# Where the networks' code stands: behind the attention's branch, or in each arm of it

## The chip, the cores and the metric

The kernel runs on one core of one Trainium2 chip. Time is the device time of one execution in microseconds. The kernel before was timed three times: 876.01, 876.82 and 877.76 us, median 876.82 us. Lower is better.

## The reference, cut to what matters

Three stages follow one another; the arrays are float32.

```python
def reference(q, k, v, n_sink, window, w_in, w_out, domain_probs, w1, w2):
    # 1 attention: batch 2, 8 heads, 768 positions, head size 64; scores q.k/8, kept where the
    #   key is one of the first n_sink or 0 <= i - j < window; softmax; times v
    x = attention.transpose(0, 2, 1, 3).reshape(1536, 512)
    # 2 first network: 512 -> 2048 -> 512
    h = x @ w_in
    x = (h * tanh(log1p(exp(min(h, 20))))) @ w_out
    # 3 second network: 4 experts, 512 -> 1024 -> 512, mixed by normalised domain_probs
    p = domain_probs / (domain_probs.sum(-1) + 1e-9)
    return sum(p[:, e:e+1] * (relu(x @ w1[e]) @ w2[e]) for e in range(4))
```

`n_sink` is 4 and `window` is 128 here, but both are inputs that the kernel reads while it runs.

## The kernel before, in words

Each engine has an instruction stream of its own, written out in the order in which it runs, and the engines meet through semaphores. Every weight and activation is split into two parts (`_hi` and `_lo`), so one product of matrices is three passes of TensorE (PE).

**The branch.** VectorE (DVE) works out a flag from `n_sink` and `window` (L1317). PE, ScalarE (ACT), DVE and GpSimd (POOL) each load it into a register and branch by it (L769, L1061, L1500, L473): where the flag is 1 they run `window_attention`, which computes only the blocks of scores near the diagonal and the sinks; otherwise `full_attention`, which computes all scores. With the inputs here every engine runs `window_attention`. The code of the other arm lies in the stream behind it and is jumped over; that jump is recorded under the line of the `If`, as its second execution. Behind the two arms, once in the stream of each engine, stands the code of both networks. The queue of SyncE (SP), which loads tiles and stores the output, has no such branch.

**The end of the attention.** `window_attention` ends with the start of the first network. On PE three `start_up` steps (L594, 12 passes each, 128x512) are laid between the last attention steps. On ACT it ends with `take_after` (L967, the copy of the last attention output to `x_hi`). On DVE it ends with its counterpart for `x_lo` (L1403). On POOL it ends with the scaling of probabilities (L443).

**The first network.** For each of 6 passes over 512 tokens (3 chunks, two groups of 8 tiles of the hidden layer) `chunk` alternates `up` (12 matmuls of L594 into one PSUM bank) and, three steps later, `down` (12 matmuls of L783). Between them stands the gate: DVE takes the bank (L1345), ACT an exponential (L945), DVE L1351, ACT a logarithm and an exponential (L949, L951), DVE four operations (L1361, L1364, L1371, L1377), ACT the high part (`gate_hi`, L1079), DVE the low part (`gate_lo`, L1514), and `down` waits for that (`mish_lo`). ACT also splits weight tiles (L958, L961), whose low part POOL completes by a DMA that adds (L439). The first thing that ACT does in the networks' code is such a split, L958; PE's first is the fourth `up`; DVE's is `gate_lo(0)`, which waits for ACT; POOL's is an add (L439), which waits for ACT. The last three passes on PE are a hardware loop (L803).

**The second network.** 16 pairs of hidden tiles by 2 halves of the tokens: `product` (L812, seven products in place of eight) and `tile_down` (L886), and DVE adds the results into the output accumulators (`evict`, L1655). Most of it is a hardware loop on every engine (L929 on PE, L1251 on ACT, L1716 on DVE). A loop's branch back is recorded under the loop's line.

**The end.** DVE's last `evict` frees the last output tile, SP stores it (L417) and waits for it to land. At L115 all five engines then meet: each drains and reports, POOL collects the reports and releases all.

Of the kernel before, what the change touches and what calls it, by code (L numbers as in the profile page):

```python
# [106 lines left out]
def build(nc, qT, kT, v, vs, params, weights, probs, out):  # L107
# [7 lines left out]
    with ExitStack() as ctx:  # L115
# [305 lines left out]
        def _(pl):  # L421
# [48 lines left out]

            pl.wait_ge(flag_ready, 1)
# [12 lines left out]

            def raw_blocks(p):
                r = 2 * (p % 2)
                return [w_raw[:, r + n, 2 * P * k:2 * P * (k + 1)] for n in range(2) for k in range(2)]

            def make_s1(p):

                for r in (2 * (p % 2), 2 * (p % 2) + 1):
                    pl.wait_ge(raw_in[r], 16 * ((FIRST + 2 * p) // RAW + 1))
                if p >= 2:
                    pl.wait_ge(w_sum_in, 16 * p)
                _, _, a21, a22 = raw_blocks(p)
                pl.tensor_tensor(sums_of(p)[:, 0, :], a21, a22, ALU.add).then_inc(w_sum_done, 1)

            def make_s2(p):
                pl.wait_ge(w_sum_done, 4 * p + 1)
                a11, _, _, _ = raw_blocks(p)  # L500
                pl.tensor_tensor(sums_of(p)[:, 1, :], sums_of(p)[:, 0, :], a11, ALU.subtract).then_inc(w_sum_done, 1)

            def make_s3(p):
                a11, _, a21, _ = raw_blocks(p)
                pl.tensor_tensor(a21, a11, a21, ALU.subtract).then_inc(w_sum_done, 1)

            def make_s4(p):
                pl.wait_ge(w_sum_done, 4 * p + 2)
                _, a12, _, _ = raw_blocks(p)
                pl.tensor_tensor(sums_of(p)[:, 2, :], a12, sums_of(p)[:, 1, :], ALU.subtract).then_inc(w_sum_done, 1)  # L510

            def add_tokens(s, name, count):

                pl.wait_ge(x_neg_done, count)
                source = rows(t_temp(s, name)) if name[0] == "T" else x2_block(s, int(name[1]) - 1, int(name[2]) - 1)
                pl.dma_start(rows(x_part(True, s, name)), source, accum_op=ALU.add).then_inc(x_added[s][name], 16)

            def add_sums(p):

                pl.wait_ge(w_neg_done, FIRST + 3 * p + (3 if p < 2 else 1))  # L520
                if p >= 1:
                    pl.wait_ge(w_sum_in, 16 * p)
                pl.dma_start(sum_cols(w_lo, p % 2), sums_of(p), accum_op=ALU.add).then_inc(w_sum_in, 16)  # L523

            def add_tile(p, n):

                r = 2 * (p % 2) + n
                pl.wait_ge(w_neg_done, FIRST + 3 * p + n + (1 if p < 2 else 2))
                pl.dma_start(w_cols(w_lo, p % 2 * SLOT + n * WC, WC), w_raw[:, r, :], accum_op=ALU.add)\
                    .then_inc(w_lo_in[r], 16)  # L530

            add_raw(EARLY - 1, (EARLY - 1) % RAW, EARLY)
            for t in range(NC * MISH):
                for f in range(STEPS):
                    for k, _ in splits(t, f):
                        add_raw(k % STEPS, k % RAW, (t // NC) * STEPS + k + 1)
            before_last, last = STEPS * (NC * MISH - 2), STEPS * (NC * MISH - 1)
            pl.wait_ge(g_done, before_last + 4)
            make_s1(0)
            pl.wait_ge(g_done, before_last + 5)  # L540
            make_s2(0)
            pl.wait_ge(g_done, before_last + 6)
            make_s3(0)
            pl.wait_ge(g_done, before_last + 7)
            make_s4(0)

            pl.wait_ge(g_done, last)
            make_s1(1)
            pl.wait_ge(g_done, last + 1)
            make_s2(1)  # L550
            pl.wait_ge(g_done, last + 2)
            make_s3(1)
            pl.wait_ge(g_done, last + 3)
            make_s4(1)
            add_tile(0, 0)
            add_tile(0, 1)
            add_tokens(0, "T1", 1)
            add_sums(0)
            add_tokens(0, "T2", 2)
            add_tokens(0, "T3", 3)  # L560
            add_tokens(0, "B22", 4)
            add_tile(1, 0)
            add_tile(1, 1)
            add_sums(1)
            add_tokens(1, "B21", 5)
            add_tokens(1, "B22", 6)

            pl.wait_ge(xc_lo, len(LO_ORDER[0]) + len(LO_ORDER[1]))
            for p in range(2, PAIRS):
                make_s1(p)  # L570
                make_s2(p)
                make_s3(p)
                make_s4(p)
                add_sums(p)
                add_tile(p, 0)
                add_tile(p, 1)

        @block.tensor
        def _(pe):
# [186 lines left out]

            pe.wait_ge(flag_ready, 1)
# [6 lines left out]
            def down(s, f, drained, by_bank=False):  # L774
                hidden_ready(s)
                g = f % G_RING
                for i in range(CT):
                    if f == 0 and drained is not None:

                        pe.wait_ge(bank_out, drained + i + 1)  # L780
                    lo, hi = CT * P + i * P, CT * P + (i + 1) * P
                    for n, (w, h) in enumerate(((w_hi, g_hi), (w_hi, g_lo), (w_lo, g_hi))):
                        mm = pe.matmul(banks[:, i, :], w[:, f, lo:hi], g_slot(h, g), start=(f == 0 and n == 0),  # L783
                                       stop=(f == STEPS - 1 and n == 2), skip_group_check=True)
                    if by_bank and i < CT - 1:
                        mm.then_inc(last_down, 1)
                mm.then_inc(down_done, 1)

            def chunk(t, c, before):
                for f in range(STEPS):  # L790
                    if before or f >= LAG:
                        up(t, c, t * STEPS + f, f, before)
                    if f >= LAG:
                        down(t * STEPS + f - LAG, f - LAG, (t - 1) * CT if before else None)
                    elif before:
                        down(t * STEPS + f - LAG, f - LAG + STEPS, None)


            pe.wait_ge(x_lo_done, X_DONE)
            chunk(0, 0, False)  # L800
            for t in range(1, NC):
                chunk(t, t, True)
            with pe.Fori(NC, NC * MISH) as t:  # L803
                chunk(t, t % NC, True)

            BANK_A, BANK_B, BANK_C = 4, 5, 7

            def product(bank, at, name, p2, s, first, last):

                for k in range(2):  # L810
                    for n, (w, lo) in enumerate(((w_hi, False), (w_hi, True), (w_lo, False))):
                        mm = pe.matmul(banks[:, bank, 0:HALF], w_cols(w, p2 * SLOT + at + k * P, P),  # L812
                                       x_part(lo, s, name)[:, k * HALF:(k + 1) * HALF],
                                       start=(first and k == 0 and n == 0), stop=(last and k == 1 and n == 2),
                                       skip_group_check=True)
                mm.then_inc(prod_done, 1)

            def tokens_ready(p, s, name):
                if isinstance(p, int) and p == 0 and name in ADDED[s]:
                    pe.wait_ge(x_added[s][name], 16)  # L820
                elif isinstance(p, int) and p == 0:
                    pe.wait_ge(xc_lo, len(LO_ORDER[0]) * s + LO_ORDER[s].index(name) + 1)

            def product_1(p, turn, p2, s):
# [116 lines left out]
        def _(act):  # L941
# [121 lines left out]
            with act.Else():  # L1063
                full_attention()
# [698 lines left out]
```

## Time and profile before

| what | value |
|---|---|
| median of 3 runs | 876.82 us |
| the profiled execution's own time | 877.44 us |
| its span, first to last instruction | 875.6 us |
| outside the span | 1.84 us |
| PE / DVE / ACT / POOL busy | 858.6 / 614.7 / 401.6 / 170.0 us |
| granted clock of TensorE | 1.00 in every slice |

The span is shown in slices of 21.9 us; PE is at 6 to 9 tenths in the first five (the attention), at 9 tenths in nearly all others. The profile's "issue" is time in which an engine stood still for nothing that the profile shows: no semaphore and no transfer.

### The profile page before, as it was taken

How to read it: one execution, taken by the hardware profiler on the slowest of the kernel's cores; microseconds unless marked ns; L12 is line 12 of the kernel's file. 1: busy time of each engine (PE TensorE's matmuls, PEld its weight loads, DVE VectorE, ACT ScalarE, POOL GpSimd, SP SyncE). 2: the span in 40 equal slices, each digit the busy share in tenths (PEclk: the TensorE clock that was granted, in tenths of full speed). 3: DMA queues.
4: the chain of work that ended last, by engine and by line, in shares of the span. 5: the costliest groups of instructions: out<-in, count | busy, mean ns of one | idle time of the engine just before them, and what ended most of it. 6: DMA issues, size and time to landing. Idle time of an engine off the chain costs nothing.

```text
span 875.6 us, 13835 instructions
## 1 busy us (share of the span) xinstructions
PE 858.6 (98%) x4448; PEld 733.5 (84%) x4448; DVE 614.7 (70%) x1219; ACT 401.6 (46%) x739; POOL 170.0 (19%) x255
## 2 busy tenths in 40 slices
PE   6999989999999999999999999999999999999998
PEld 4666767888888888889989999889998899998897
DVE  5888759989898999985665655656566565565655
ACT  4878755444874455873233133134224313313410
POOL 4666510000110011221220122022022112202100
PEclk9999999999999999999999999999999999999999
DMA  7454642000681000780541352254055135313303
GB/s 250 126 132 115 155 108 66 0 1 1 133 203 49 0 0 6 164 167 1 115 102 34 93 114 49 64 114 87 26 114 114 28 86 114 58 56 66 66 1 144
DMA packets 25192, 72.72 MB, mean 83 GB/s; under 512 B 4288, under 2 KB 5952, under 8 KB 25152
## 3 DMA queue, kind: packets, MB, share of 16 engines
q0 software_dynamic: 10720, 33.82, 21.2%
q1 hardware_dynamic: 14288, 38.04, 13.2%
q10 hardware_dynamic: 144, 0.39, 0.2%
q8 instruction: 17, 0.28, 0.1%
q14 instruction: 23, 0.19, 0.1%
HBM read 35.28 MB, written 3.15 MB: 44 GB/s over the span
## 4 chain that ended last, share of the span: by engine, by line
PE 92%; ACT 3%; DVE 2%; issue 1%; DMA 0%; DVEq 0%; POOL 0%; ACTq 0%
PE banks L886 30%; PE banks L812 27%; PE banks L783 14%; PE banks L594 14%; PE banks L609 2%; PE banks L680 2%; ACT pool L972 2%; PE banks L650 2%; PE banks L661 1%; DMA prm<-params 0%; ACT pool L949 0%; DVE g_lo L1514 0%; DVE pool L1423 0%; ACT w_hi L958 0%; ACT pool L951 0%
## 5 line engine op out<-in xcount | busy, mean ns | idle before, releaser
L1655 DVE SCALAR_TENSOR_TENSOR pool<-banks,p_norm,pool 128x512 f32<-128x512 f32 x180 | 133.6, 749 | 66.6 <-PE banks L886 64.8
L886 PE MATMUL banks<-w_hi,g_lo 128*128 128x512 f32 x384 | 150.6, 392 | 0.0
L886 PE MATMUL banks<-w_lo,g_hi 128*128 128x512 f32 x384 | 150.5, 392 | 0.0
L886 PE MATMUL banks<-w_hi,g_hi 128*128 128x512 f32 x384 | 149.3, 389 | 0.0
L1196 ACT ACTIVATE g_hi<-pool 128x384 fp32r<-128x384 f32 x96 | 50.5, 526 | 190.8 <-DVE pool L1635 139.2
L812 PE MATMUL banks<-x_hi,w_lo 128*128 128x384 f32 x256 | 85.9, 336 | 0.0
L812 PE MATMUL banks<-x_hi,w_hi 128*128 128x384 f32 x256 | 85.9, 335 | 0.0
L812 PE MATMUL banks<-x_lo,w_hi 128*128 128x384 f32 x256 | 85.7, 335 | 0.0
L886 PEld LDWEIGHTS banks<-w_hi,g_lo 128*128 128x128 f32 x384 | 72.1, 188 | 15.1
L886 PEld LDWEIGHTS banks<-w_lo,g_hi 128*128 128x128 f32 x384 | 72.1, 188 | 13.9
L886 PEld LDWEIGHTS banks<-w_hi,g_hi 128*128 128x128 f32 x384 | 72.1, 188 | 13.6
L783 PE MATMUL banks<-g_hi,w_hi 128*128 128x512 f32 x192 | 75.6, 394 | 1.8 <-DVE g_lo L1514 1.8
L594 PE MATMUL banks<-x_hi,w_hi 128*128 128x512 f32 (+1 forms) x192 | 75.1, 391 | 1.4 <-issue 1.4
L1190 ACT ACTIVATE g_hi<-banks 128x384 fp32r<-128x384 f32 x32 | 15.7, 491 | 131.3 <-PE banks L812 131.3
L523 POOL DMA_DIRECT2D w_lo<-w_sum x15 | 13.1, 875 | 323.2 <-ACT w_lo L1106 323.2
L783 PE MATMUL banks<-g_hi,w_lo 128*128 128x512 f32 x192 | 74.8, 390 | 0.0
L783 PE MATMUL banks<-g_lo,w_hi 128*128 128x512 f32 x192 | 74.8, 390 | 0.0
L594 PE MATMUL banks<-x_hi,w_lo 128*128 128x512 f32 (+1 forms) x192 | 74.7, 389 | 0.0
L594 PE MATMUL banks<-x_lo,w_hi 128*128 128x512 f32 (+1 forms) x192 | 74.7, 389 | 0.0
L1642 DVE SCALAR_TENSOR_TENSOR g_lo<-pool,g_hi 128x384 fp32r<-128x384 f32 x96 | 53.3, 556 | 21.6 <-ACT g_hi L1196 17.8
L949 ACT ACTIVATE pool<-pool,two 128x512 f32<-128x512 f32 x48 | 34.8, 725 | 70.0 <-DVE pool L1351 69.9
L443 POOL TENSOR_TENSOR pool<-pool,row_den 128x272 f32<-128x272 f32 (+2 forms) x96 | 54.6, 594 | 39.2 <-DVE row_den L1396 39.0
(134 smaller groups left out, 1752.0 us busy)
## 6 DMA issues: line engine op xcount, KB each, us to landing
w_raw<-weights SPq DMA_DIRECT2D x48, 512.0 KB, 4.3
w_lo<-w_raw POOLq DMA_DIRECT2D x48, 512.0 KB, 5.4
w_lo<-w_sum POOLq DMA_DIRECT2D x15, 384.0 KB, 4.0
pool<-kT SPq DMA_DIRECT2D x8, 400.0 KB, 4.4
pool<-v SPq DMA_DIRECT2D x8, 384.0 KB, 3.2
out<-pool SPq DMA_DIRECT2D x12, 256.0 KB, 2.0
pool<-qT SPq DMA_DIRECT2D x7, 384.0 KB, 3.2
w_lo<-pool POOLq DMA_DIRECT2D x2, 384.0 KB, 4.9
```

What stands on the lines that cost most here:

```text
L443: pl.tensor_tensor(p, p, inverse.to_broadcast([P, width]), ALU.mult).then_inc(prob_ready, 1)
L594: mm = pe.matmul(banks[:, 4 + f % H_RING, :], w[:, f, k * P:(k + 1) * P], x[:, k, ds(c * CHUNK, CHUNK)], start=(k == 0 and n == 0), stop=( ...
L609: mm = pe.matmul(bank[:, col:col + n], q_pair[rows, b, j * P:(j + 1) * P], k_pair[rows, b, key:key + n], start=True, stop=True)
L650: mm = pe.transpose(banks[:, TURN_BANK + n, P * (2 * h + k):P * (2 * h + k) + P], window_prob(u + h, WIDE)[:, col:col + P], ident[:, :])
L680: mm = pe.matmul(banks[D * h:D * h + D, out_bank, column], v_pair[:, b, kt, D * h:D * h + D], prob_T[:, slot, P * (2 * h + k):P * (2 * h + ...
L783: mm = pe.matmul(banks[:, i, :], w[:, f, lo:hi], g_slot(h, g), start=(f == 0 and n == 0), stop=(f == STEPS - 1 and n == 2), skip_group_che ...
L812: mm = pe.matmul(banks[:, bank, 0:HALF], w_cols(w, p2 * SLOT + at + k * P, P), x_part(lo, s, name)[:, k * HALF:(k + 1) * HALF], start=(fir ...
L886: mm = pe.matmul(banks[:, bank, :], g[:, s, f * SUP + at:f * SUP + at + P], w_cols(w, p2 * SLOT + DOWN_AT[f], DM), start=(f == 0 and n == ...
L949: act.activation(r_buf[:, s % 2, :], n_buf[:, s % 2, :], ACT.Ln, bias=two[:, 0:1]).then_inc(l_done, 1)
L1196: act.activation(relu_of(s, f, l), source, ACT.Relu).then_inc(relu_hi, 1)
L1642: dve.scalar_tensor_tensor(out=g_lo[:, s, at], in0=source, scalar=0.0, in1=g_hi[:, s, at].bitcast(f32), op0=ALU.max, op1=ALU.subtract).the ...
L1655: dve.scalar_tensor_tensor(out=to, in0=d_bank, scalar=share, in1=to, op0=ALU.mult, op1=ALU.add)\
```

## The change

On each of the four engines that branch, everything that stood behind the two arms (both networks, with their loops) becomes a function `networks()`, and that is called at the end of each arm. The body of `networks()` is what stood there, line by line, with a deeper indent. SP's stream is not changed, nor are the waits, the tiles and the order on any engine. Each stream now has the code of the networks twice; the one that lies in the other arm isn't run. GpSimd's part in full but for the body, and the other three by their branches:

```diff
@@ gpsimd
+            def networks():
+                def raw_blocks(p):
...
+                add_raw(EARLY - 1, (EARLY - 1) % RAW, EARLY)
...
             pl.wait_ge(flag_ready, 1)
             small = pl.value_load(flag[0:1, 0:1])
             with pl.If(small == 1):
                 window_attention()
+                networks()
             with pl.Else():
                 pl.iota(prob[:, 0, :], ...
                 full_attention()
-            def raw_blocks(p):
...
-            add_raw(EARLY - 1, (EARLY - 1) % RAW, EARLY)
...
+                networks()
@@ tensor
             with pe.If(small == 1):
                 window_attention()
+                networks()
             with pe.Else():
                 full_attention()
+                networks()
@@ scalar
             with act.If(small == 1):
                 window_attention()
+                networks()
             with act.Else():
                 full_attention()
+                networks()
@@ vector
             with dve.If(small == 1):
                 window_attention()
+                networks()
             with dve.Else():
...
                 full_attention()
                 steps[0] = before
+                networks()
```

So the jump over the other arm, which stood between the attention and the networks, now stands between the last instruction of the networks and the meeting at L115.

## Rows read from the trace of the kernel before

**Rows 1.** The page's head and part 1: busy time, share, instructions.
```profile
span 875.6 us, 13835 instructions
PE 858.6 (98%) x4448; PEld 733.5 (84%) x4448; DVE 614.7 (70%) x1219; ACT 401.6 (46%) x739; POOL 170.0 (19%) x255
```

**Rows 2.** Waits, 112 to 136 us: engine, line, releaser, us, times, longest.
```profile
ACT w_hi L958 <- issue: 4.0, 1, 4.0
...
PE banks L783 <- DVE g_lo L1514: 1.6, 3, 0.8
PE banks L594 <- issue: 1.4, 1, 1.4
```

**Rows 3.** Branches by source line: ns min/median/max, first and last start.
```profile
L769 PEldq COMPARE_BRANCH  x2: 80/2421/4762, 7.3 to 111.7; - x2
...
L1061 ACTq COMPARE_BRANCH  x2: 40/44/47, 7.1 to 112.4; - x2
...
L1500 DVEq COMPARE_BRANCH  x2: 47/48/50, 8.5 to 112.8; - x2
...
L473 POOLq COMPARE_BRANCH  x2: 38/42/45, 7.1 to 104.3; - x2
```

**Rows 4.** Timeline of ACT: start us, us, engine, line, operation, idle before.
```profile
112.37 0.39 ACT L967 ACTIVATE x_hi<-banks 128x256 fp32r<-128x256 f32 x1 [3.34 <-PE banks L680]
116.70 1.06 ACT L958 ACTIVATE w_hi<-w_raw 128x1024 fp32r<-128x1024 f32 x1 [3.95 <-issue]
```

**Rows 5.** DMA queues, 112 to 116 us: packets, MB, share of 16 engines.
```profile
q8 instruction: 2, 0.03, 4.5%
q14 instruction: 2, 0.02, 1.6%
```

**Rows 6.** Timeline of POOL.
```profile
105.03 0.88 POOL L439 DMA_DIRECT2D w_lo<-w_raw  x1 [0.47 <-ACT w_lo L961]
```

**Rows 7.** Timeline of DVE.
```profile
119.27 0.69 DVE L1514 TENSOR_TENSOR g_lo<-pool,g_hi 128x512 fp32r<-128x512 f32 x1 [6.06 <-ACT g_hi L1079]
```

**Rows 8.** Timeline of PE around the end of the attention.
```profile
112.25 0.50 PE L594 MATMUL banks<-x_hi,w_hi 128*128 128x512 f32 x1
...
116.71 0.47 PE L594 MATMUL banks<-x_hi,w_hi 128*128 128x512 f32 x1 [1.42 <-issue]
...
132.82 0.50 PE L783 MATMUL banks<-g_hi,w_hi 128*128 128x512 f32 x1 [0.75 <-DVE g_lo L1514]
```

**Rows 9.** The chain of waits: start us, us, what.
```profile
132.07 0.70 DVE g_lo L1514
...
138.57 2.72 PE banks L783 x12
```

**Rows 10.** Stretches: length, busy by engine (count), clock, DMA share, GB/s.
```profile
136.00:160.00 24.00, 24.00 (x108) 19.87 (x107) 23.14 (x43) 12.57 (x21) 0.00 (x0) 1.00 0.05 18
...
480.00:840.00 360.00, 360.00 (x1804) 325.50 (x1803) 213.43 (x349) 117.05 (x183) 61.91 (x79) 1.00 0.35 77
```

**Rows 11.** Source line L115, the meeting at the end, columns as in rows 3.
```profile
L115 PEldq DRAIN  x1: 4267/4267/4267, 868.1 to 868.1; - x1
L115 DVEq DRAIN  x1: 789/789/789, 872.4 to 872.4; - x1
...
L115 SPq DRAIN  x1: 13/13/13, 875.4 to 875.4; - x1
```

**Rows 12.** Loop branches by source line, columns as in rows 3.
```profile
L803 PEldq COMPARE_BRANCH  x3: 76/216/247, 273.6 to 360.8; - x3
...
L929 PEldq COMPARE_BRANCH  x7: 76/208/211, 471.0 to 844.7; - x7
...
L1716 DVEq COMPARE_BRANCH  x7: 50/56/80, 476.1 to 849.9; - x7
```

**Rows 13.** DMA queues, 475 to 730 us: all that moved.
```profile
q0 software_dynamic: 3562, 11.86, 25.7%
q1 hardware_dynamic: 2304, 8.39, 9.8%
```

More of the change, by code:

```diff
@@ L469, in full_attention, with make_s1, make_s2, make_s3 @@
                     add_raw(k, k, k + 1)
+            def networks():
+                def raw_blocks(p):
+                    r = 2 * (p % 2)
+                    return [w_raw[:, r + n, 2 * P * k:2 * P * (k + 1)] for n in range(2) for k in range(2)]
+                def make_s1(p):
+                    for r in (2 * (p % 2), 2 * (p % 2) + 1):
+                        pl.wait_ge(raw_in[r], 16 * ((FIRST + 2 * p) // RAW + 1))
+                    if p >= 2:
+                        pl.wait_ge(w_sum_in, 16 * p)
+                    _, _, a21, a22 = raw_blocks(p)
+                    pl.tensor_tensor(sums_of(p)[:, 0, :], a21, a22, ALU.add).then_inc(w_sum_done, 1)
+                def make_s2(p):
+                    pl.wait_ge(w_sum_done, 4 * p + 1)
+                    a11, _, _, _ = raw_blocks(p)
+                    pl.tensor_tensor(sums_of(p)[:, 1, :], sums_of(p)[:, 0, :], a11, ALU.subtract).then_inc(w_sum_done, 1)
+                def make_s3(p):
+                    a11, _, a21, _ = raw_blocks(p)
+                    pl.tensor_tensor(a21, a11, a21, ALU.subtract).then_inc(w_sum_done, 1)
+                def make_s4(p):
+                    pl.wait_ge(w_sum_done, 4 * p + 2)
+                    _, a12, _, _ = raw_blocks(p)
+                    pl.tensor_tensor(sums_of(p)[:, 2, :], a12, sums_of(p)[:, 1, :], ALU.subtract).then_inc(w_sum_done, 1)
+                def add_tokens(s, name, count):
+                    pl.wait_ge(x_neg_done, count)
+                    source = rows(t_temp(s, name)) if name[0] == "T" else x2_block(s, int(name[1]) - 1, int(name[2]) - 1)
+                    pl.dma_start(rows(x_part(True, s, name)), source, accum_op=ALU.add).then_inc(x_added[s][name], 16)
+                def add_sums(p):
+                    pl.wait_ge(w_neg_done, FIRST + 3 * p + (3 if p < 2 else 1))
+                    if p >= 1:
+                        pl.wait_ge(w_sum_in, 16 * p)
+                    pl.dma_start(sum_cols(w_lo, p % 2), sums_of(p), accum_op=ALU.add).then_inc(w_sum_in, 16)
+                def add_tile(p, n):
+                    r = 2 * (p % 2) + n
+                    pl.wait_ge(w_neg_done, FIRST + 3 * p + n + (1 if p < 2 else 2))
+                    pl.dma_start(w_cols(w_lo, p % 2 * SLOT + n * WC, WC), w_raw[:, r, :], accum_op=ALU.add)\
+                        .then_inc(w_lo_in[r], 16)
+                add_raw(EARLY - 1, (EARLY - 1) % RAW, EARLY)
+                for t in range(NC * MISH):
+                    for f in range(STEPS):
+                        for k, _ in splits(t, f):
+                            add_raw(k % STEPS, k % RAW, (t // NC) * STEPS + k + 1)
+                before_last, last = STEPS * (NC * MISH - 2), STEPS * (NC * MISH - 1)
+                pl.wait_ge(g_done, before_last + 4)
+                make_s1(0)
+                pl.wait_ge(g_done, before_last + 5)
+                make_s2(0)
+                pl.wait_ge(g_done, before_last + 6)
+                make_s3(0)
+                pl.wait_ge(g_done, before_last + 7)
+                make_s4(0)
+                pl.wait_ge(g_done, last)
+                make_s1(1)
+                pl.wait_ge(g_done, last + 1)
+                make_s2(1)
+                pl.wait_ge(g_done, last + 2)
+                make_s3(1)
+                pl.wait_ge(g_done, last + 3)
+                make_s4(1)
+                add_tile(0, 0)
+                add_tile(0, 1)
+                add_tokens(0, "T1", 1)
+                add_sums(0)
+                add_tokens(0, "T2", 2)
+                add_tokens(0, "T3", 3)
+                add_tokens(0, "B22", 4)
+                add_tile(1, 0)
+                add_tile(1, 1)
+                add_sums(1)
+                add_tokens(1, "B21", 5)
+                add_tokens(1, "B22", 6)
+                pl.wait_ge(xc_lo, len(LO_ORDER[0]) + len(LO_ORDER[1]))
+                for p in range(2, PAIRS):
+                    make_s1(p)
+                    make_s2(p)
+                    make_s3(p)
+                    make_s4(p)
+                    add_sums(p)
+                    add_tile(p, 0)
+                    add_tile(p, 1)
@@ L483, in _ @@
                 full_attention()
-            def raw_blocks(p):
[L486 to L496, printed above, removed]
@@ L512, in add_tokens @@
[L512 to L523, printed above, removed]
@@ L525, in add_tile @@
[L525 to L530, printed above, removed]
-            add_raw(EARLY - 1, (EARLY - 1) % RAW, EARLY)
[L533 to L550, printed above, removed]
@@ L568, in _ @@
[L568 to L576, printed above, removed]
+                networks()
         @block.tensor
@@ L770, in _ @@
                 window_attention()
+                networks()
             with pe.Else():
                 full_attention()
[L774 to L824, printed above, removed]
-                it = 2 * p + s
-                if not isinstance(it, int) or it >= 1:
-                    pe.wait_ge(relu_lo, 4 * it - 3)
-                pe.wait_ge(w_lo_in[2 * p2], 16 * turn + 16)
-                tokens_ready(p, s, "B11")
-                product(BANK_A, A11, "B11", p2, s, True, False)
@@ L935, in _ @@
-            final = PAIRS - 1
-            pair_step(final, (FIRST + 2 * final) // RAW, 1, 1, final, 1)
-            for k in range(SUP_TILES):
-                tile_down(final, 1, 1, k)
+                networks()
         @block.scalar
@@ L1081, in x_hi_of @@
-            def x_hi_of(s, name):
-                if name[0] == "T":
-                    act.wait_ge(t_made, 4 * s + T_ORDER[s].index(name) + 1)
-                    act.wait_ge(up_done, STEPS * (NC * MISH - 1 + s))
-                    source = rows(t_temp(s, name))
-                else:
-                    if s == 0:
-                        act.wait_ge(bank_out, CT * (NC + 2 if name == "B22" else NC + 1))
-                    else:
-                        act.wait_ge(bank_out, CT * (NC * MISH - 1) + 2 * int(name[1]))
-                        act.wait_ge(down_done, NC * MISH * STEPS)
-                    source = x2_block(s, int(name[1]) - 1, int(name[2]) - 1)
-                act.activation(rows(x_part(False, s, name)), source, ACT.Copy).then_inc(xc_hi, 1)
@@ L1096, in x_neg_of @@
-            def x_neg_of(s, name):
-                source = rows(t_temp(s, name)) if name[0] == "T" else x2_block(s, int(name[1]) - 1, int(name[2]) - 1)
-                act.activation(rows(x_part(True, s, name)), source, ACT.Copy, scale=-1.0).then_inc(x_neg_done, 1)
-            def sums_hi(p, p2):
-                act.wait_ge(w_sum_done, 4 * p + 4)
-                act.activation(sum_cols(w_hi, p2), sums_of(p), ACT.Copy)
-            def sums_neg(p, p2):
-                act.activation(sum_cols(w_lo, p2), sums_of(p), ACT.Copy, scale=-1.0).then_inc(w_neg_done, 1)
@@ L1192, in relu_sum @@
-            def relu_sum(it, s, n):
-                f, l, source = ((1, 1, c22), (0, 1, c12), (1, 0, c21))[n - 1]
-                act.wait_ge(sum_done, 5 * it + 2 + n)
-                act.activation(relu_of(s, f, l), source, ACT.Relu).then_inc(relu_hi, 1)
-            def relus(it, s):
-                relu_first(it, s)
-                for n in range(1, 4):
-                    relu_sum(it, s, n)
-            def next_weights(p, turn, p2):
-                act.wait_ge(tile_done, 2 * SUP_TILES * p - 2 * SUP_TILES)
-                sums_hi(p, p2)
-                sums_neg(p, p2)
-                tile_hi(p, turn, p2, 0)
-                tile_neg(p2, 0)
@@ L1266, in _ @@
-            for s in range(2):
-                copy_p1(2 * PAIRS - 2 + s)
-                relus(2 * PAIRS - 2 + s, s)
+                networks()
         @block.vector
@@ L1545, in x_lo_of @@
-            def x_lo_of(s, name):
-                dve.wait_ge(xc_hi, BLOCKS * s + HI_ORDER[s].index(name) + 1)
-                if s == 1 and name[0] == "T":
-                    dve.wait_ge(w_sum_in, 32)
-                source = rows(t_temp(s, name)) if name[0] == "T" else x2_block(s, int(name[1]) - 1, int(name[2]) - 1)
-                dve.tensor_tensor(rows(x_part(True, s, name)), source, rows(x_part(False, s, name)).bitcast(f32),
-                                  ALU.subtract).then_inc(xc_lo, 1)
@@ L1598, in _ @@
-            gate_lo(NC * MISH * STEPS - 2)
-            finish_first(NC * MISH * STEPS - 1)
-            finish_second(NC * MISH * STEPS - 1)
-            def bank(n):
-                return banks[:, n, 0:HALF]
-            def halves_used(it, n):
-                if not isinstance(it, int) or it >= 1:
-                    dve.wait_ge(relu_lo, 4 * it - 4 + n)
-            def sum_16(it, s):
-                halves_used(it, 3)
-                dve.wait_ge(prod_done, 7 * it + (3 if isinstance(it, int) and it == 0 else 2))
-                dve.wait_ge(p1_copied, it + 1)
-                dve.tensor_tensor(c12, bank(5 + s), p1_sum, ALU.add).then_inc(sum_done, 1)
@@ L1645, in evict @@
-            def evict(it, s, e, first, k):
-                dve.wait_ge(tile_done, SUP_TILES * it + k + 1)
-                tile = TILE_ORDER[k]
-                to, d_bank = out_acc(s, tile), banks[:, (2 * s + k) % 4, :]
-                token = s * SUP_TILES + tile
-                share = p_norm[:, ds(e, 1), token:token + 1].rearrange("p a n -> p (a n)")
-                if first:
-                    dve.tensor_scalar(to, d_bank, share, None, ALU.mult).then_inc(evicted, 1)
-                else:
-                    dve.scalar_tensor_tensor(out=to, in0=d_bank, scalar=share, in1=to, op0=ALU.mult, op1=ALU.add)\
-                       .then_inc(evicted, 1)
@@ L1721, in _ @@
-            pair_step(2 * PAIRS - 1, 1, E - 1, False)
-            for k in range(SUP_TILES):
-                evict(2 * PAIRS - 1, 1, E - 1, False, k)
+                networks()
 def kernel(q, k, v, n_sink, window, moe_w_in, moe_w_out, moe2_domain_probs, moe2_w1, moe2_w2):
```

920 lines of the change are left out of this document (510 added, 410 removed).

## The prediction

> **What bounds the kernel now.** Read in this order: the busy shares, the waits around the end of the attention, the branch records, the timelines of ACT and PE there, and last the meeting at the end. PE is busy for 858.6 of 875.6 us, and from 136 us on it never stands still (24.00 us busy of 24.00, later 360.00 of 360.00) [rows 1, 10]. [...] So any microsecond that the change takes from a standstill of PE before 136 us moves all later work forward as a whole, and one put on PE behind that is paid in full.
>
> Between 112 and 136 us PE has two kinds of standstill: 1.4 us of "issue" ahead of the fourth `up`, and three waits for `gate_lo`, 1.6 us together. ACT has one "issue" idle of 4.0 us in the same place [rows 2]. The branch records explain both. ACT reaches its jump over the other arm at 112.4 us, and the record lasts only 47 ns, but the next ACT instruction starts at 116.70 us, with nothing to wait for: 3.95 us of idle behind a copy that began at 112.37 us [rows 3, 4]. PE reaches its jump at 111.7 us and that record itself lasts 4.76 us, to 116.46 us; PE had a queue of matmuls to work off and shows only the last 1.42 us of it [rows 3, 8]. In these four microseconds the instruction queues move four packets [rows 5]. So the jump makes an engine fetch its next code, and costs it about 4.3 us (ACT, 112.4 to 116.70) to 4.8 us (PE).
>
> [...]
>
> **The part taken away.** Behind `window_attention` the next instruction now follows in sequence, so ACT starts L958 at about 112.75 in place of 116.70 us, 3.95 us earlier. Does PE gain as much? DVE's `gate_lo(0)` waited 6.06 us for ACT and nothing else [rows 7], so the whole chain of gates moves with ACT. The last wait of PE ends at 132.82 us; what released it was DVE L1514 at 132.07 us, itself released by ACT's high part [rows 8, 9], and that chain would end 3.95 us earlier: 128.87 us. PE's own work allows that: from 112.25 to 132.82 us it has six groups of twelve matmuls, a group that waits for nothing takes 2.72 us [rows 9], so 16.3 us plus 0.1 for the start of the first: 128.7 us, 4.1 us earlier [rows 8]. The later of the two counts: **gain 3.95 us**. PE's first `up` itself comes 1.4 us earlier, its first `down` no longer waits, and the third `down` is the one late by 0.2 us.
> Bounds: at least the 3.0 us of standstill that the waits show (1.4 + 1.6) [rows 2], at most the 4.1 us of PE's own work. I take 3.95, as the gates limit. Nothing else is late: POOL's add and SP's loads wait for ACT and follow it. DVE's own jump, at 112.8 us, lies under the wait for ACT (its next record is at 119.27) and is worth nothing by itself [rows 3, 7]. POOL's jump, at 104.3 us, was cheap: its next operation starts at 105.03, 0.7 us later, of which 0.47 us is a wait [rows 3, 6].
>
> **The part added.** Each of the four engines now jumps over the other arm, which has become longer by the networks, ahead of its drain at L115. The cost is what the latest of them adds to the meeting. PE is at its drain at 868.1 us, with 4.27 us of matmuls still queued, to 872.4 us; SP is last, at 875.4 us [rows 11]. With a jump of 4.8 us PE is there by 872.9 us: hidden. ACT and POOL have less to do for the last pair than PE and are ahead of it: hidden. DVE is not hidden: its drain is issued at 872.4 us, when its last `evict` starts, 3.0 us ahead of SP's [rows 11]. With a jump of J in between, the meeting is J - 3.0 us later. DVE's jump in this trace is only bounded: below by POOL's 0.7 us, above by 119.27 - 112.8 = 6.5 us [rows 3, 6, 7]. The nearest rows are ACT's 4.3 and PE's 4.8 us; I take 4.5, so **cost 1.5 us**, with ends 0 (J under 3.0, SP's last store covers it) and 3.5 us.
>
> **Loops and the rest.** The networks' code moves in each stream, and the loops stand elsewhere against the pieces in which code is fetched. Here the branch back costs PE about 0.21 us, under a full queue, and DVE 0.06 us [rows 12], and between 475 and 730 us no instruction packet moves at all [rows 13]: all loop bodies stay held. I price the shift at nothing, as the cover for it (held code) doesn't depend on where in a piece a loop begins, so far as its body is held with room to spare; if it isn't, that is rival C. Waits, tiles and transfers are unchanged; the second copy of the code isn't run and costs only its place.
>
> **Sum.** 877.44 (the profiled execution; span 875.6 and 1.84 around it) - 3.95 + 1.5 = 874.99 us. That execution lies 0.62 us above the median of the three runs, 876.82, so the median to expect is 874.4 us, 2.45 us or 0.28% lower. The least that a measurement of this kernel can tell from no change is about 0.2%, 1.75 us. The forecast's own range: gain 4.1, cost 0: 872.7; gain 3.0, cost 3.5: 877.3.
>
> **The rivals.**
> - A, the end is free: DVE's jump hides under the last store. That wants J under 3.0 us. For: POOL's jump cost 0.7 us at most. Against: POOL jumped over a short arm, DVE jumps over a whole copy of attention and networks. 876.82 - 3.95 = 872.9 us.
> - B, the gain is only PE's own: ACT's idle is not the jump's, or the gates turn late by something else, and only the 1.42 us of PE's "issue" goes, while the end still pays 1.5. For: one trace, one jump per engine, and "issue" is a name for what isn't seen. Against: ACT's and PE's idle have one time and one length, and PE's is in the branch record itself [rows 3, 4]. 876.9 us. With it stands the case that the jump never cost anything and nothing changes: 876.8 us.
> - C, slower: a loop that was held is held no more after the shift, and PE fetches at each branch back. There are 8 taken ones (2 of the 3 records of L803, 6 of the 7 of L929) [rows 12]. Each would be a fetch as at the jump, of which PE's queue left 1.42 us showing [rows 8]: 8 x 1.42 = 11.4 us, 874.4 + 11.4 = 885.8 us. It decides from 0.5 us per turn on, where it eats 2.45 + 1.75 us. For: the code does shift. Against: rows 12 and 13, loops of very different lengths held on PE and DVE.
> - D, the end costs twice: behind the meeting the engines run on, outside the span, in code that was prefetched in sequence and that after a jump must be fetched once more; another 4.3 us in place of nothing: 878.7 us. For: 1.84 us outside the span that no row explains. Against: after ACT's jump at 112.4 us no second gap follows [rows 2].
>
> [...]
>
> **How the numbers follow.** Forecast 0.62, A 0.10, B with no change 0.13, C 0.06, D 0.09. Faster by over 0.2% means under 875.07: four fifths of the forecast (J up to about 5.1) and all of A, 0.60. B and the rest of the forecast are within 0.2%, 0.25. C and D are slower, 0.15. The range that leaves out C, the upper half of D and the very edge of A is 872.6 to 878.2 us.
>
> **What would show it.** In the changed kernel's profile: no "issue" idle ahead of ACT L958 and PE L594 near 112 us; ACT's L958 starts within 0.1 us of the end of L967; the last wait of PE for `gate_lo` ends at about 128.9 us; all later PE groups are 3.95 us earlier, and DVE's last `evict` starts at 868.4 us. A branch record of DVE then stands there, its drain comes at about 872.9 us and SP's at 871.4, so DVE, not SP, is last at L115; the span is about 873.1 us. Wrong it would be if PE's branch-back records grew above 0.3 us, if instruction packets appeared in the loops, or if DVE's drain came within 3.0 us of the last `evict` (A) or more than 5.1 us behind it.

## The result, and the profile after

| | before | after |
|---|---|---|
| median of 7 runs each (lowest to highest) | 876.82 us (876.01 to 877.76) | 874.23 us (873.23 to 874.49) |
| ratio | | 0.9971, interval 0.9961 to 0.9981 |
| the profiled execution, its span | 877.44, 875.6 us | 874.49, 872.7 us |
| outside the span | 1.8 us | 1.8 us |

The change makes the kernel 2.6 us (0.29%) faster; 874.4 us was forecast. In the profile it is 4.1 us gained behind the attention and 1.2 us given back at the end. The second of these has another cause than the one forecast.

The lines of the kernel have shifted with the edit: the branches are L939 (PE), L1272 (ACT), L1724 (DVE), L567 (POOL); `up` is L597, `down` L780, the splits L964 and L967, the copy of x L973, `gate_lo` L1511, `evict` L1652.

First, page head and busy times of after [rows 1]:

```profile
span 872.7 us, 13835 instructions
PE 857.5 (98%) x4448; PEld 733.7 (84%) x4448; DVE 614.7 (70%) x1219; ACT 401.4 (46%) x739; POOL 170.0 (19%) x255
```

Where the 4.1 us come from: the waits of after between 112 and 136 us [rows 2] have no `issue` idle of ACT any more and none of PE before a matmul, only one of 0.2 us before a weight load.

```profile
ACT x_hi L973 <- PE banks L683: 3.3, 1, 3.3
DVE g_lo L1511 <- ACT g_hi L1079: 2.0, 1, 2.0
PEld banks L780 <- DVE g_lo L1511: 0.3, 1, 0.3
PEld banks L597 <- issue: 0.2, 1, 0.2
```

The timelines of ACT, DVE and PE of after in the same place (start us, length us, engine, line, operation, idle before it) [rows 4, 7, 8]:

```profile
112.37 0.39 ACT L973 ACTIVATE x_hi<-banks 128x256 fp32r<-128x256 f32 x1 [3.34 <-PE banks L683]
112.65 1.05 ACT L964 ACTIVATE w_hi<-w_raw 128x1024 fp32r<-128x1024 f32 x1
...
115.20 0.69 DVE L1511 TENSOR_TENSOR g_lo<-pool,g_hi 128x512 fp32r<-128x512 f32 x1 [1.99 <-ACT g_hi L1079]
...
112.25 0.50 PE L597 MATMUL banks<-x_hi,w_hi 128*128 128x512 f32 x1
115.13 0.39 PE L597 MATMUL banks<-x_hi,w_hi 128*128 128x512 f32 x1
...
128.76 0.50 PE L780 MATMUL banks<-g_hi,w_hi 128*128 128x512 f32 x1
```

The copy of the last x begins at 112.37 us in both profiles, so these rows compare directly. ACT's first split starts 4.05 us sooner (116.70 to 112.65), the fourth `up` 1.58 us sooner, and the third `down`, the last that waited before, 4.06 us sooner (132.82 to 128.76) and with no wait. From there the gain is carried to the end: DVE's last `evict` waits for PE as before and starts 4.09 us sooner (872.40 to 868.31).

```profile
868.31 0.75 DVE L1652 SCALAR_TENSOR_TENSOR pool<-banks,p_norm,pool 128x512 f32<-128x512 f32 x1 [0.61 <-PE banks L883]
```

The jump itself is where it was put: each branch's second record is now at the end [rows 3]. The view is that of the branch records by source line (ns shortest/middle/longest, first and last start in us); with them the drains of L115 [rows 11].

```profile
L939 PEldq COMPARE_BRANCH  x2: 89/1984/3880, 7.4 to 864.1; - x2
L1272 ACTq COMPARE_BRANCH  x2: 38/42/45, 7.2 to 860.8; - x2
L1724 DVEq COMPARE_BRANCH  x2: 47/48/50, 8.5 to 868.3; - x2
...
L115 ACTq DRAIN  x1: 80/80/80, 863.4 to 863.4; - x1
L115 PEldq DRAIN  x1: 328/328/328, 868.0 to 868.0; - x1
L115 DVEq DRAIN  x1: 71/71/71, 871.5 to 871.5; - x1
L115 SPq DRAIN  x1: 13/13/13, 872.5 to 872.5; - x1
```

A jump's price is read as the drain's start less the branch's: ACT 2.6 us, DVE 3.2 us, PE 3.9 us. DVE reaches its drain at 871.5 us, ahead of SP: it is not last. SP is, as before, but 1.2 us later than its work should allow: from the last `evict` to the end of the span it is 3.2 us before (872.40 to 875.6) and 4.4 us after (868.31 to 872.7). What grew is the landing of the last store. Its issue in the stretch 869 to 873 us of after (queues: packets, MB, share of 16 engines; then the issue, KB, us to landing), and behind the dots the stretch 870.9 to 872.0 us alone:

```profile
q1 hardware_dynamic: 211, 0.37, 24.8%
q8 instruction: 1, 0.02, 1.5%
q14 instruction: 2, 0.02, 1.0%
...
out<-pool SPq DMA_DIRECT2D x1, 256.0 KB, 3.2
...
DMA  0100100100200100100100100100101000000000
...
q1 hardware_dynamic: 14, 0.02, 5.4%
```

The same stretch around the last store of the kernel before, 873 to 876 us:

```profile
q1 hardware_dynamic: 226, 0.40, 35.4%
...
out<-pool SPq DMA_DIRECT2D x1, 256.0 KB, 2.0
```

The store takes 3.2 us in place of 2.0, and in its last microsecond packets of the store alone move, one after the other, at the tenths that one of 16 DMA engines gives: fifteen are done and one is late. That it is one DMA engine is read from the share (5.4% of 16 engines) and the even spacing; the trace doesn't name the engine. The new company of the store is the code that PE fetches when it resumes behind its jump (868.0 us): one packet of 16 KB on q8, which by its record starts at 869.22 us and takes 0.98 us, as long as twelve of the store's packets of 2 KB (0.08 us each). Two packets of 8 KB on q14, DVE's by their time, move there too (869.6 and 872.1 us); e3 and e5 tell the two apart.

The loops are as before [rows 10, 12, 13]: branch back and stretches of after (length, busy by engine, clock, DMA share, GB/s).

```profile
L926 PEldq COMPARE_BRANCH  x7: 76/215/228, 466.9 to 840.7; - x7
L1713 DVEq COMPARE_BRANCH  x7: 50/56/69, 472.0 to 845.8; - x7
...
480.00:830.00 350.00, 350.00 (x1755) 316.54 (x1754) 207.12 (x339) 114.40 (x179) 59.12 (x76) 1.00 0.35 77
```

### The profile page after: what moved, and what is told of

Read it like the earlier page. It is cut to its first block, busy times and chain, and to the rows that moved or that the text cites. A ratio compares the mean times of both kernels' runs of the same rounds, so it can differ in the third digit from the quotient of the medians.

```text
span 872.7 us, 13835 instructions
## 1 busy us (share of the span) xinstructions
PE 857.5 (98%) x4448; PEld 733.7 (84%) x4448; DVE 614.7 (70%) x1219; ACT 401.4 (46%) x739; POOL 170.0 (19%) x255
## 3 DMA queue, kind: packets, MB, share of 16 engines
HBM read 35.28 MB, written 3.15 MB: 44 GB/s over the span
## 4 chain that ended last, share of the span: by engine, by line
PE 96%; ACT 1%; DVE 1%; issue 1%; DMA 1%; POOL 0%; DVEq 0%; ACTq 0%
PE banks L883 30%; PE banks L809 27%; PE banks L780 15%; PE banks L597 15%; PE banks L612 3%; PE banks L683 2%; PE banks L653 2%; ACT pool L978 1%; PE banks L664 1%; DMA prm<-params 1%; DVE pool L1432 0%; DVE mask L1303 0%; DVE pool L1392 0%; PE banks L651 0%; POOL pool L443 0%
## 5 line engine op out<-in xcount | busy, mean ns | idle before, releaser
L1652 DVE SCALAR_TENSOR_TENSOR pool<-banks,p_norm,pool 128x512 f32<-128x512 f32 x180 | 133.6, 749 | 66.7 <-PE banks L883 64.9
L780 PE MATMUL banks<-g_hi,w_hi 128*128 128x512 f32 x192 | 75.3, 392 | 0.2 <-DVE g_lo L1511 0.2
L597 PE MATMUL banks<-x_hi,w_hi 128*128 128x512 f32 (+1 forms) x192 | 75.0, 391 | 0.0
L780 PE MATMUL banks<-g_hi,w_lo 128*128 128x512 f32 x192 | 74.8, 390 | 0.0
L780 PE MATMUL banks<-g_lo,w_hi 128*128 128x512 f32 x192 | 74.8, 389 | 0.0
L597 PE MATMUL banks<-x_hi,w_lo 128*128 128x512 f32 (+1 forms) x192 | 74.7, 389 | 0.0
L597 PE MATMUL banks<-x_lo,w_hi 128*128 128x512 f32 (+1 forms) x192 | 74.7, 389 | 0.0
```

The source lines that it names most:

```text
L597: mm = pe.matmul(banks[:, 4 + f % H_RING, :], w[:, f, k * P:(k + 1) * P], x[:, k, ds(c * CHUNK, CHUNK)], start=(k == 0 and n == 0), stop=( ...
L1652: dve.scalar_tensor_tensor(out=to, in0=d_bank, scalar=share, in1=to, op0=ALU.mult, op1=ALU.add)\
```

## The experiments

Each kernel's time stands against the kernel before in the same series (its medians there: 876.41 for e1, e2, e3 and e5, 876.62 for e4 and e6 to e8, 876.67 for e9 to e11). The end of the attention falls up to a microsecond earlier or later from run to run (the copy of the last x at 111.4 to 113.4 us in these profiles), so the profiles are split at two points that don't depend on it. **Way**: from the start of that copy to the start of the last `evict`. **Tail**: from there to the end of the span. The last store is given from its issue to its landing. Each kernel has one profile, so way, tail and store are one execution's.

| kernel | way, us | tail, us | last store, us | median | less before | ratio, interval |
|---|---|---|---|---|---|---|
| before | 760.03 | 3.2 | 2.0 | 876.82 | | |
| after | 755.94 | 4.4 | 3.2 | 874.23 | -2.59 | 0.9971, 0.9961 to 0.9981 |
| e11, after again | 755.98 | 4.3 | 3.2 | 874.17 | -2.50 | 0.9975, 0.9966 to 0.9985 |
| e1, ACT only | 757.67 | 3.2 | 2.0 | 874.30 | -2.11 | 0.9975, 0.9963 to 0.9986 |
| e2, PE only | 758.47 | 3.7 | 2.5 | 876.76 | +0.35 | 1.0001, 0.9992 to 1.0010 |
| e3, DVE and POOL | 759.60 | 3.4 | 2.2 | 876.59 | +0.18 | 1.0000, 0.9991 to 1.0009 |
| e4, all but PE | 757.77 | 3.3 | 2.1 | 874.94 | -1.68 | 0.9981, 0.9972 to 0.9990 |
| e5, PE and ACT | 756.46 | 4.5 | 3.3 | 874.74 | -1.67 | 0.9980, 0.9971 to 0.9989 |
| e6, hint late | 758.63 | 3.2 | 2.0 | 875.70 | -0.92 | 0.9989, 0.9980 to 0.9998 |
| e7, hint late, DVE too | 758.47 | 3.2 | 2.0 | 875.62 | -1.00 | 0.9988, 0.9979 to 0.9997 |
| e8, after, PE's end hinted | 755.99 | 3.4 | 2.3 | 873.47 | -3.15 | 0.9962, 0.9948 to 0.9975 |
| e9, and DVE's end | 755.95 | 3.4 | 2.2 | 874.10 | -2.57 | 0.9974, 0.9963 to 0.9985 |
| e10, before, hint early | 756.23 | 3.2 | 2.0 | 873.39 | -3.28 | 0.9963, 0.9950 to 0.9977 |

The profiled execution of before was 0.62 us above its median. If that excess lies in its way and tail, they overstate a gain against the medians by as much; with it taken off, the two agree within 0.4 us in all but e2 and e9 (by 0.8 and 0.7 us). The intervals of the ratios are some 1 us wide to each side, so differences of 1 us or less between two of the kernels are read from the profiles and not from the medians.

Theory 1, after the two traces: the way is ACT's and PE's jump, and the tail is PE's code fetch in the way of the last store. Theory 2: the tail is DVE's jump, as forecast, or DVE's fetch.

**e1, e2 and e3: one engine's part alone.** The networks stay behind the branch on the engines that are not named; on them, as here on PE for e1:

```diff
             with pe.If(small == 1):
                 window_attention()
-                networks()
             with pe.Else():
                 full_attention()
-                networks()
+            networks()
```

> The networks stand inside the arms on ACT alone; PE, DVE and POOL as before. Theory 1 (the gates set the gain, and at the end PE's code fetch delays the last store): PE keeps its jump and resumes at 116.7 us, then runs five groups without a wait, so its third down starts at 116.71 + 2.83 + 4 x 2.72 = 130.4 in place of 132.82 us, 2.4 us earlier, and the end costs nothing: 876.8 - 2.4 = 874.4 us, last store landed in 2.0 us. Theory 2 (DVE's jump is what costs at the end) gives the same here. Rival 3 (each engine's idle counts by itself, PE's 1.4 and ACT's remainder 2.6): 874.2 us.

> The networks stand inside the arms on PE alone. Theory 1: PE's fourth up starts 1.6 us earlier, but the gates wait for ACT's jump as before, the third down stays at 132.8 us, nothing is gained; at the end PE's code fetch meets the last store, which lands in 3.2 in place of 2.0 us: 876.8 + 1.2 = 878.0 us. Theory 2 (DVE's jump costs at the end): 876.8 us. Rival 3 (PE's own idle counts by itself): 1.4 us less at the start, 875.4 us, with or without 1.2 at the end.

> The networks stand inside the arms on DVE and POOL alone. Theory 1: nothing at the start (both jumps lie under waits), and at the end DVE's drain comes 3.15 us after its last evict, about when SP's does: 876.8 to 877.0 us, last store landed in 2.0 us. Theory 2: DVE's code fetch delays the last store: 878.0 us with a landing of 3.2 us.

e1 came at -2.1 us, with the tail of before: ACT's part alone carries most of the gain and nothing of the cost. What it leaves is PE's own idle, 1.5 us here.

```profile
PE banks L597 <- issue: 1.5, 1, 1.5
```

e2 was expected 1.2 us above before and came level, a miss. Its way is 1.6 us shorter though ACT still jumps: where PE doesn't jump, ACT's jump is shorter too. The timeline of ACT in e2 and the third `down` of PE:

```profile
115.11 1.06 ACT L964 ACTIVATE w_hi<-w_raw 128x1024 fp32r<-128x1024 f32 x1 [2.34 <-issue]
...
131.22 0.50 PE L780 MATMUL banks<-g_hi,w_hi 128*128 128x512 f32 x1 [0.75 <-DVE g_lo L1511]
```

ACT starts 2.7 us after the jump in place of 4.3. At the end PE's code packet (871.14 us, 1.06 us long) ends 1.3 us after the last `evict` begins, against 1.7 to 2.0 us in after, e11 and e5: here it meets the store before the last, which takes 3.2 us, and the last one takes 2.5. So what PE's jump costs at the end depends on where its fetch falls. That the median shows none of the 1.6 us beside a tail that is only 0.5 us longer is not explained by this profile.

e3 is the test of theory 2. DVE's jump is at the end, PE's is not; DVE's drain comes 0.1 us ahead of SP's, and the tail grows by 0.2 us, not by 1.2:

```profile
L115 DVEq DRAIN  x1: 70/70/70, 875.1 to 875.1; - x1
L115 SPq DRAIN  x1: 13/13/13, 875.2 to 875.2; - x1
```

DVE's jump of 3.1 us just fits under the last store, and the 0.2 us are the store's own (2.2 us in place of 2.0), with DVE's packet of 8 KB 0.6 us ahead of its first packet. Theory 2 falls as the account of the 1.2 us. DVE's own jump at the start was worth little beside the others: the way is 0.4 us shorter, with ACT's idle 3.60 in place of 3.95 us, and the median shows nothing.

**e5 and e4: what the parts do together.** The same edit, with PE and ACT inside, and with all but PE inside.

> The networks stand inside the arms on PE and ACT, not on DVE and POOL. Theory 1: the whole gain of 4.06 us at the start, and PE's code fetch still delays the last store by 1.2 us: 876.8 - 4.06 + 1.2 = 873.9 us, as with all four engines. Theory 2: the gain without the cost, 872.8 us, last store landed in 2.0 us. Both: the third down of PE at 128.8 us.

> The networks stand inside the arms on ACT, DVE and POOL, not on PE. PE resumes behind its own jump at 116.5 us or up to 1.6 us sooner, if the fetches of ACT and DVE are what lengthens it; then five groups without a wait. With PE's jump unchanged at 4.8 us: third down at 130.4, 2.4 us gained, and at the end only DVE's jump of 3.1 us, which ends with SP's drain: 876.4 - 2.4 + 0.1 = 874.1 us. If the end's cost were DVE's: 875.3 us.

In e5 the tail is the longest of all (4.5 us, last store 3.3 us, PE's fetch at 868.99 us taking 1.76 us), with DVE's jump not at the end at all: PE's part brings it without DVE's. The median, 874.7 us, is 0.8 us above the 873.9 expected. At the start DVE's jump now shows: it takes 2.8 us (112.7 to 115.55 us), `gate_lo(0)` is 0.35 us later than in after, and the third `down` waits for it again, 0.29 us:

```profile
129.11 0.50 PE L780 MATMUL banks<-g_hi,w_hi 128*128 128x512 f32 x1 [0.29 <-DVE g_lo L1511]
```

So the jump that was worth next to nothing with ACT's in place is worth 0.4 us without it: it is the next delay behind ACT's. In e4 PE jumps alone and takes 5.0 us, 1.7 of it past its queue; the other engines' jumps are not what makes PE's long. The tail is 3.3 us without PE's jump in it. The median, 874.9 us, is 0.8 us above the 874.1 expected.

**e8 and e11: the code fetched ahead.** The hint of these kernels gives a branch an earlier place in the stream (`mark_branch_hint_location`, `branch_hint`); that the fetch of its target can begin there was the author's assumption, and what it does is read from the runs (PE's jump at the end takes 3.9 us in after and 0.46 us in e8). e8 is the changed kernel with such a hint for PE's jump at the end, ahead of its last six `tile_down`; e11 is the changed kernel as it is.

```diff
+                hint_at[0] = pe.mark_branch_hint_location()
                 for k in range(SUP_TILES):
...
             with pe.If(small == 1):
+                behind = nc.cur_bb.bb.name.replace("_true", "_end")
                 window_attention()
                 networks()
+                pe.br(behind).branch_hint(hint_at[0])
```

> The changed kernel with a prefetch hint on PE's jump at the end, placed ahead of its last six output tiles. Theory 1 (PE's second fetch, at 869.2 us, delays the last store by sharing one DMA engine with it): PE jumps without a stall near 864 us, its fetches lie before 867 us, the last store lands in 2.0 us, and the end costs nothing: 0.5 to 1.2 us below the changed kernel, 872.4 us where before is 876.4. Theory 2 (DVE's fetch at 869.6 us delays it): landing stays at 3.2 us, no gain, 873.8 us.

> The changed kernel once more, in one job with its two relatives. All theories: 0.3% below before (0.2 to 0.4%), last store landed in 2.5 to 3.3 us, third down of PE 16.5 us after the first start_up pass of the third start_up.

PE's jump at the end falls from 3.9 to 0.46 us. Its two code packets start at 861.3 and 866.3 us, so none moves during the jump (865.1 us), and none is under the last store, whose packets are done after 2.3 us. The branch of PE in e8:

```profile
L945 PEldq COMPARE_BRANCH  x1: 457/457/457, 865.1 to 865.1; - x1
```

The tail is 3.4 us, against 4.3 and 4.4 us in the two profiles of the changed kernel: the cost of the tail is gone, with PE's jump and its fetch moved and nothing else changed. A store of 3.1 us is still there (the longest of the twelve), near the packet at 866.3 us, but it isn't the last. The median is 0.65 us further below the kernel before than e11's; the two intervals overlap, and it missed the 872.4 us expected by 1.1.

**e9: DVE's jump hinted too.** The same edit again on DVE, ahead of its loop over the second network.

> The changed kernel with hints on the end jumps of PE and of DVE. Theory 1: with PE's late fetch gone the last store lands in 2.0 us and SP would reach the meeting 3.0 us behind DVE's last evict; DVE's jump of 3.1 us is then as late as SP, so its hint is worth at most 0.2 us beside PE's hint alone. The whole 4.06 us of the start stay: 0.95 to 1.2 us below the changed kernel in this job, about 0.4% below the kernel before. If the end's cost had another source, equal to the changed kernel.

DVE's jump shrinks to 0.64 us, its drain comes 2.5 us ahead of SP's, and the tail stays at 3.4 us, as it must where SP is last. The median came out with e11's and not with e8's, a miss (0.95 to 1.2 us below the changed kernel was expected), though the profiled execution itself was at 873.37 us. So the tail is shown by the profiles; that the medians gain by it is not shown.

**e6 and e7: the hint on the kernel before, ten microseconds ahead.** No code is copied; the jump behind the attention gets the hint, on PE ahead of `start_up(0)` and on ACT ahead of its last splits in the attention; in e7 on DVE ahead of `start_gate(0)` too.

> The kernel before, its code not copied; PE and ACT get a prefetch hint for their jump over the other arm, some ten microseconds ahead of it. If the whole price of the jump is the fetch of its target, ACT's idle of 3.95 and PE's of 1.42 us go, with only DVE's own jump left (gate_lo late by 0.3 to 0.4 us, as where PE and ACT alone had the networks inside), and nothing is added at the end: 876.4 - 3.7 = 872.7 us. If the jump costs by itself, whatever has been fetched, no change: 876.4 us.

> As e6_hint, with the hint on DVE's jump too. Fetch theory: the whole 4.06 us of the start and no cost at the end, 876.4 - 4.06 = 872.3 us, last store landed in 2.0 us, which is below both kernels. If the jump costs by itself: 876.4 us.

Both missed, by 3.0 and 3.3 us. No packet of PE's code moved ahead of the jump. Yet the hint did something: PE's jump takes 3.0 us in place of 4.8, ACT's 2.9 and 2.7 us in place of 4.3, the way is 1.4 to 1.6 us shorter, and the median 0.9 to 1.0 us lower. What went is one packet of PE's code: 16 of 16 KB in the whole execution in place of 17, and one in place of two right behind the jump (before: 112.33 and 112.77 us; e6: 112.03 us). A packet of 16 KB moves at this place in the kernels without a jump of PE there as well (112.48 us in after, 112.42 in e2), and such packets move where PE runs on without a gap (before: 152.50 and 181.92 us, with PE busy for 104.00 of 104.00 us from 136 us on). So the first of before's two is likely a fetch in sequence, of code that is then jumped over, and the jump's own comes behind it. That reading was not tested by itself.

**e10: the same hint, far earlier.** On PE and DVE it is the first thing in the arm, on ACT it stands about 45 us ahead of the jump.

```diff
             with pe.If(small == 1):
+                behind = nc.cur_bb.bb.name.replace("_true", "_end")
+                hint_at = [pe.mark_branch_hint_location()]
                 window_attention()
+                pe.br(behind).branch_hint(hint_at[0])
...
+                        if ct == CT - 2 and g == 3:
+                            hint_at[0] = act.mark_branch_hint_location()
```

> The kernel before, no code copied, with the hints on the jump behind the attention placed far ahead: on PE and DVE as the first instruction of the arm, on ACT some 70 instructions earlier than in e6_hint. There the hints brought no fetch ahead of the jump; if that was because no new piece of code was fetched between hint and jump, the targets are now fetched early, the jumps cost under 0.5 us and the start's whole 4.06 us are gained without any cost at the end: 0.46% below before. If a fetched target is dropped again before the jump, or a hint ahead of a loop has no effect: as e6_hint, 0.1% below before.

ACT goes on 0.5 us after its jump, 0.2 us later than with no jump at all; PE's still takes 3.2 us, not under 0.5 as expected, but that lies under its queue. ACT's timeline and PE's branch in e10:

```profile
112.22 0.38 ACT L976 ACTIVATE x_hi<-banks 128x256 fp32r<-128x256 f32 x1 [3.35 <-PE banks L683]
112.72 1.06 ACT L967 ACTIVATE w_hi<-w_raw 128x1024 fp32r<-128x1024 f32 x1
...
L943 PEldq COMPARE_BRANCH  x1: 3211/3211/3211, 111.5 to 111.5; - x1
```

The way is 3.8 us shorter and the tail that of before: 873.39 us, the lowest median of all, 0.8 us under the changed kernel's in the same series (the intervals overlap), with the networks' code once in each stream. Against e8 (873.47 us, in another series) it is no different by these runs.

## Why the prediction was right

- **What bounds the kernel, and the gain of 3.95 us:** right; 4.06 us at the third `down` and 4.09 at the last `evict`. Of the two counts that were set against each other, PE's own work (4.1 us) was the one that held in the end: `gate_lo` was in time, and the third `down` has no wait. That ACT's jump is the larger part and PE's 1.4 us the smaller is e1's result.
- **The jump's price of 4.3 to 4.8 us:** right for the gaps it was read from, wrong as the price of a jump. ACT's is 2.7 us in e2 and 2.6 at the end of after, DVE's 2.8 in e5 and 2.9 to 3.2 at the end (e4, e3, after), PE's 3.8 (e2) and 3.9 at the end. Where two packets of PE's code move close together, ACT's is 4.0 to 4.3 us (e3, before), DVE's 4.0 (e1) and PE's own 4.8 to 5.0, alone too (e4).
- **DVE's J of 4.5 us, so 1.5 us at the end:** the term that was mis-sized. J is 3.2 us, so DVE's drain is 1.0 us ahead of SP's in place of 1.5 behind it, and 0.1 us ahead where PE doesn't jump (e3); DVE's part costs at most 0.2 us by itself, and that through the store (2.2 us in e3). POOL's 0.7 us, the lower bound that was given, was no price of a jump over the arm: its next operation starts at 105.05 us in after, with no jump, as against 105.03 before, and at the end its jump takes 3.8 us (820.6 to its drain at 824.4).
- **PE's jump at the end is hidden:** the step that failed. PE's drain is indeed early (868.0 us), but the cover was reckoned for the engine and not for the DMA that its jump starts. The fetch (0.98 us at 869.22 us) lies, by the reading of its packets above, in front of the last store's on one DMA engine, and the store is 1.2 us late. Shown by the store of 2.0 us in e1 and no more than 2.2 us in e3 and e4 (no PE jump at the end), 3.2 and 3.3 us in e11 and e5 (with it), and 2.3 us in e8 (with it, fetched early). In e2 the jump is there and the store takes 2.5 us, as the fetch falls earlier.
- **So the sum was right partly by luck:** 1.5 us for a reason that costs 0.2 stood in for 1.2 us of a reason priced at nothing. Without the second the sum gives rival A's 872.9 us. The profiles of e8 and e9 bear that out (way and tail together 3.8 us shorter than before's); their medians do so only in part (3.15 and 2.57 us lower, so 873.7 and 874.2 us against 876.82).
- **DVE's own jump at the start is worth nothing by itself:** right as said, within the 0.4 us by which e3's way is shorter; 0.4 us once ACT's is gone (e5), and the change has both.
- **POOL at nothing, loops at nothing (C), nothing behind the meeting (D):** right; branches back 215 and 56 ns, no instruction packet between 480 and 730 us, 1.8 us outside the span in both. That code is fetched ahead in sequence, as D has it, is seen on PE inside the span (packets at 152.50 and 181.92 us of before, under a PE without a gap); behind the meeting no trace shows it. B falls with e1.

## What to carry to other kernels

A branch over a long arm cost its engine 2.5 us (ACT at the end of e5) to 3.9 us (PE at the end of after) here, and up to 5.0 us (PE in e4) where two packets of PE's code moved at once, so look at what each engine is late for behind its jump, and price each with the others in place and with them gone. A jump that is hidden for its engine still moves code (16 KB at 869.2 us in after): look which transfer near it is the last one of the kernel. A hint far ahead of the branch gave at least the same gain here without a second copy of the code (e10: 873.39 us, e11: 874.17 us). Whether one worked is read from the gap behind the branch, engine by engine: packets of code ahead of it move with and without a hint (861.3 us in e8, 860.2 us in after).

## What the runs showed of the hardware that was not expected

- PE's jump is longer where two fetches of its code lie close together: it takes 4.8 to 5.0 us behind the attention in before, e1, e3 and e4, with two packets of 16 KB within 0.5 us that take 1.0 to 1.9 us each, and 3.0 to 3.2 us in e6, e7 and e10, where the second comes 3.0 to 3.6 us later. The eight packets of these pairs take 1.54 us on average; the other 208 of this size in the thirteen profiles take 1.09 (median 0.98, longest 1.90, in e1 at 122.4 us), and one beside the last stores takes 1.76 (e5). The hinted kernels move one packet of 16 KB less in all (16 against 17); that the first of the two is a fetch in sequence past the branch would fit, and stays untested.
- By their times, PE's code moves on q8 in packets of 16 KB (a late one, at 871.1 us, in e2, where PE jumps at the end; none behind 846.7 us in e3, where it doesn't); those seen behind the jumps of ACT, DVE and POOL are of 8 KB on q14, 0.3 to 0.6 us each. DVE's go with a slightly longer last store: it takes 2.1 to 2.3 us in e3, e4, e8 and e9, with a packet of 8 KB 0.3 to 0.6 us ahead of its first, and 2.0 us in before, e1, e6, e7 and e10, with none there.
- A hint 10 us ahead of the jump brought no early fetch (e6 and e7: no packet of 16 KB between 49.9 and 111.3 us), though it shortened the jumps, and one far ahead cut ACT's jump from 4.3 to 0.5 us (e10) and DVE's at the end to 0.64 (e9). PE's with six `tile_down` between (e8) fell to 0.46 us, and with the whole attention between (e10) only to 3.2, as with the late hint (3.0). The condition for an early fetch in e10's expectation, a new piece of code fetched between hint and jump, was not shown: in e10 packets of 16 KB moved at 22, 36 and 50 us, between the two, and PE's jump still took 3.2 us. What a hint wants stays open.
